# Attention and two mixtures of experts in one kernel: a different order of the first loads, scalings and casts

## What is computed

```
gamma = 1.0 - 2.0 ** (-5.0 - arange(H)); scale = 1.0 / sqrt(D)
for t in range(S):
    state = gamma * state + einsum('bhd,bhe->bhde', k[:, :, t], v[:, :, t])
    y[:, :, t] = scale * einsum('bhd,bhde->bhe', q[:, :, t], state)
```

```
h = x @ w_in                                       # 512 -> 2048
x = (max(h, 0) + alpha * min(h, 0)) @ w_out        # 2048 -> 512
```

## Time and profile before

| what | value |
|---|---|
| median of 3 runs | 981.75 us (981.25 to 981.96) |
| profiled execution, its own time | 981.86 us |
| its span, first to last instruction | 979.9 us |
| TensorE matmul busy | 956.0 us (98%) |
| VectorE, ScalarE, GpSimd busy | 577.8, 255.2, 239.2 us |
| mean granted TensorE clock | 0.998 |

### The profile page before, as it was taken

The page is one execution under the profiler, slowest core; times in us unless marked ns, Lnnn a source line. Parts: engine busy times, 40 slices in busy tenths (PEclk is TensorE's granted clock), DMA queues, the critical chain, the costliest instruction groups (busy, mean ns, idle before and its releaser), DMA issues.

```text
span 979.9 us, 16519 instructions
## 1 busy us (share of the span) xinstructions
PE 956.0 (98%) x5444; PEld 792.8 (81%) x5445; DVE 577.8 (59%) x1078; ACT 255.2 (26%) x404; POOL 239.2 (24%) x192
## 2 busy tenths in 40 slices
PE   8999999999999999999999999999999999999996
PEld 7888888888888888888887888878788788787785
DVE  4656589647964697469845987664333632423531
ACT  4222121112111111121111312332433533323531
POOL 4443123331433142414341224120000000000000
PEclk9999999999999999999999999999999999999999
DMA  8431392033002300140012123355331451423311
GB/s 287 166 131 55 119 386 101 0 115 101 0 0 86 128 0 0 47 146 1 1 44 93 70 87 110 105 169 220 129 130 52 181 225 43 170 82 116 113 41 53
DMA packets 27121, 100.47 MB, mean 103 GB/s; under 512 B 4383, under 2 KB 4767, under 8 KB 22448
## 3 DMA queue, kind: packets, MB, share of 16 engines
q1 hardware_dynamic: 19280, 80.90, 23.2%
q0 software_dynamic: 4336, 12.61, 3.3%
q10 hardware_dynamic: 3456, 6.32, 2.3%
HBM read 87.19 MB, written 24.20 MB: 114 GB/s over the span
## 4 chain that ended last, share of the span: by engine, by line
PE 90%; issue 3%; DVE 2%; ACT 2%; ACTq 1%; DMA 1%; SPq 0%; DVEq 0%; POOL 0%; POOLq 0%
PE bank L676 27%; PE bank L694 27%; PE bank L801 13%; PE bank L769 11%; PE bank L572 2%; PE bank L784 2%; PE bank L618 2%; PE bank L588 2%; ACT weights_split L1370 1%; PE bank L605 1%; PE bank L661 1%; DMA en_all<-in_qk 1%; DVE attention L887 1%; DVE en_all L1138 0%; ACT scratch L1399 0%
## 5 line engine op out<-in xcount | busy, mean ns | idle before, releaser
L676 PE MATMUL bank<-activations_split,weights_split 128*128 128x512 f32 x1152 | 277.6, 391 | 0.4 <-issue 0.4
L694 PE MATMUL bank<-weights_split,activations_split 128*128 128x512 f32 x1152 | 276.1, 389 | 0.0
L694 PEld LDWEIGHTS bank<-weights_split,activations_split 128*128 128x128 f32 x1152 | 216.1, 188 | 44.9
L676 PEld LDWEIGHTS bank<-activations_split,weights_split 128*128 128x128 f32 x1152 | 215.1, 188 | 45.9 <-issue 1.5
L1511 POOL TENSOR_TENSOR activations_split<-scratch,activations_split 128x512 fp32r<-128x512 f32 x84 | 116.9, 1391 | 327.2 <-ACT activations_split L1290 319.8
L1290 ACT CAST activations_split<-scratch 128x512 fp32r<-128x512 f32 x96 | 59.8, 623 | 412.1 <-DVE scratch L927 412.1
L801 PE MATMUL bank<-weights_split,activations_split 128*128 (+1 forms) x648 | 161.5, 398 | 2.8 <-issue 1.8
L769 PE MATMUL bank<-weights_split,activations_split 128*128 (+1 forms) x648 | 153.3, 391 | 0.1
L769 PEld LDWEIGHTS bank<-weights_split,activations_split 128*128 128x128 f32 x648 | 121.0, 188 | 25.2 <-issue 0.5
L801 PEld LDWEIGHTS bank<-weights_split,activations_split 128*128 128x128 f32 x648 | 117.8, 188 | 26.4 <-issue 2.6
L986 DVE SCALAR_TENSOR_TENSOR attention<-rows,en_all 128x512 f32<-128x512 f32 x140 | 135.0, 1005 | 0.0
(11 more groups left out here) (183 smaller groups left out, 667.1 us busy)
## 6 DMA issues: line engine op xcount, KB each, us to landing
attention<-in_w_exp SPq DMA_DIRECT2D x24, 1024.0 KB, 4.9
attention<-in_kv SPq DMA_DIRECT2D x43, 256.0 KB, 3.7
expert_rows<-in_pad_rows SPq DMA_DIRECT2D x8, 1028.0 KB, 18.4
en_all<-in_w_exp SPq DMA_DIRECT2D x8, 1024.0 KB, 7.2
rows<-in_w_mlp SPq DMA_DIRECT2D x14, 512.0 KB, 3.3
rows<-expert_rows ACTq DMA_DIRECT2D x24, 257.0 KB, 2.9
attention<-in_qk SPq DMA_DIRECT2D x12, 512.0 KB, 4.7
scratch<-in_qk SPq DMA_DIRECT2D x10, 512.0 KB, 3.7
```

The lines of the kernel that those rows point to most:

```text
L676: last = mm(H_ps[f % 2][:, :], win(a, kc, f), x[:, kc, :], start=(k == 0), stop=(k == 3 * KC - 1))
L694: last = mm(bank[j][:, :], x[f % 2][:, j * P:(j + 1) * P], wout(a, f), start=(f == 0 and a == 0 and part_ == "hi"), stop=(f == FB - 1 and ...
```

## The change

SP now issues the four q/k slabs directly behind the first masks, and then the weight slabs. The four v slabs and the mask rest are issued from ScalarE's queue, ahead of everything else that ScalarE does. The q of pair 1 is scaled on VectorE, between `masked(0, 0)` and `masked(0, 1)`, and announced by a semaphore of its own; GpSimd scales pairs 2 and 3 only. In chunk 0 each pair has a result bank of its own (banks 2, 1, 0, 3), so `values(0, 2)` and `values(0, 3)` no longer wait for an `x_low`. VectorE runs `masked(0, 3)` without an `x_low` behind it, and then `x_low(0, 2)` and `x_low(0, 3)`; `x_low(0, 1)` stays ahead of `masked(0, 3)`. ScalarE's order becomes `first_values(2)`, `first_values(3)`, `split_w(0)`, `x_high(0, 1)`, `x_high(0, 2)`, `x_high(0, 3)`. Ten dummies instead of twelve.

```diff
--- before.py
+++ after.py
@@ -257,8 +257,13 @@
 
     A_ps = pair[:, :].rearrange("p (h b c) -> p h b c", h=2, b=B)
     A0_ps = [[A_ps[:, 0], A_ps[:, 1]], [b3(6), b3(7)]]
+    Y_first = [b3(2), b3(1), b3(0), b3(3)]
     Y_ps, SU_ps, SU0_ps = [b3(2), b3(1)], b3(3, D), [b3(6, D), b3(7, D)]
     H_ps = [bank[4], bank[5]]
+
+    def Y_of(c, hp):
+        return Y_first[hp] if isinstance(c, int) and c == 0 else Y_ps[hp % 2]
+
     LG_ps = bank[7][:, 0:B * E].rearrange("p (b e) -> p b e", b=B)
     RK_ps = bank[6][:, 0:B * E].rearrange("p (b e) -> p b e", b=B)
     RK_last = bank[3][:, 0:B * E].rearrange("p (b e) -> p b e", b=B)
@@ -297,7 +302,7 @@
     s_vs_first, s_q_first, s_wlo_pool, s_zero, s_tau, s_masks_rest = sem("vs_first"), sem("q_first"), sem("wlo_pool"), sem("zero"), sem("tau"), sem("masks_rest")
     s_k_ld = [sem(f"k_ld{i}") for i in range(2)]
     s_v_ld = [sem(f"v_ld{i}") for i in range(3)]
-    s_v_first = sem("v_first")
+    s_v_first, s_q_second = sem("v_first"), sem("q_second")
     s_wld = [sem(f"wld{i}") for i in range(4)]
     s_whi, s_wlo = sem("whi"), sem("wlo")
     s_vs, s_qs, s_A, s_m, s_Yi, s_SU, s_Y, s_S, s_xh, s_xl = (
@@ -440,16 +445,9 @@
 
 
             sp.dma_start(C[:, :QD + P], consts[:, :QD + P]).then_inc(s_masks, 16)
-            load_qk(0, 0)
-            load_v(0, 0)
-            sp.dma_start(C[:, QD + P:MASKS], consts[:, QD + P:MASKS]).then_inc(s_masks_rest, 16)
-            load_qk(0, 1)
-            load_v(0, 1)
-            load_qk(0, 2)
-            load_v(0, 2)
-            load_qk(0, 3)
+            for hp in range(HP):
+                load_qk(0, hp)
             load_w(0)
-            load_v(0, 3)
             load_w(1)
             sp.dma_start(alpha_sb[:, :], alpha[:, :]).then_inc(s_small, 16)
             load_w(2)
@@ -557,8 +555,10 @@
                 first = isinstance(c, int) and c == 0
                 if first and hp == 0:
                     pe.wait_ge(s_q_first, due(s_q_first, 1))
+                elif first and hp == 1:
+                    pe.wait_ge(s_q_second, due(s_q_second, 1))
                 else:
-                    pe.wait_ge(s_qs, due(s_qs, u))
+                    pe.wait_ge(s_qs, due(s_qs, u - 1))
                 if not first:
                     pe.wait_ge(s_m, due(s_m, u))
                 elif hp >= 2:
@@ -610,12 +610,10 @@
                 pe.wait_ge(s_m, due(s_m, u + 1))
                 scaled(c, hp)
                 mixed = Am_first[hp % 2] if first else Am
-                if first and hp >= 2:
-                    pe.wait_ge(s_xl, due(s_xl, u - 1))
                 for b in range(B):
                     for hh in range(2):
                         cols = slice(hh * D, (hh + 1) * D)
-                        last = mm(Y_ps[hp % 2][cols, b, :], v_sb(c, hp)[:, b, cols], mixed[:, hh, b, :],
+                        last = mm(Y_of(c, hp)[cols, b, :], v_sb(c, hp)[:, b, cols], mixed[:, hh, b, :],
                                   start=first, stop=(first or b == B - 1))
                 last.then_inc(s_Y, 1)
 
@@ -722,7 +720,7 @@
                         x_transpose(0, 1)
 
             pe.wait_ge(s_zero, due(s_zero, 1))
-            for _ in range(12):
+            for _ in range(10):
                 mm(bank[0][:, 0:P], idle_in, idle_in, start=True, stop=True)
             scores(0, 0)
             values(0, 0, first=True)
@@ -878,7 +876,7 @@
             def x_low(c, hp):
                 u = 4 * c + hp
                 dve.wait_ge(s_xh, due(s_xh, u + 1))
-                ve.tensor_tensor(x_lo[:, hp, :].rearrange("p (b c) -> p b c", b=B), Y_ps[hp % 2],
+                ve.tensor_tensor(x_lo[:, hp, :].rearrange("p (b c) -> p b c", b=B), Y_of(c, hp),
                                  x_hi[:, hp, :].rearrange("p (b c) -> p b c", b=B).bitcast(f32),
                                  ALU.subtract).then_inc(s_xl, 1)
 
@@ -902,15 +900,23 @@
                           .then_inc(s_S, 1)
                 x_low(c, HP - 1)
 
-            def first_attention():
+            def second_query():
+                dve.wait_ge(s_masks_rest, due(s_masks_rest, 16))
+                dve.wait_ge(s_qk_ld[1], due(s_qk_ld[1], 16))
+                ve.tensor_tensor(qT(0, 1), qT(0, 1), qdecay[:, 1:2, :].broadcast_to([P, B, P]), ALU.mult).then_inc(s_q_second, 1)
+
+            def first_attention(between):
                 for hp in range(HP):
                     dve.wait_ge(s_A, due(s_A, hp + 1))
                     if hp >= 2:
                         dve.wait_ge(s_Y, due(s_Y, hp - 1))
                     masked(0, hp, A0_ps[hp % 2], Am_first[hp % 2])
-                    if hp:
+                    if hp == 0:
+                        between()
+                    elif hp < HP - 1:
                         x_low(0, hp - 1)
-                x_low(0, HP - 1)
+                for hp in range(HP - 2, HP):
+                    x_low(0, hp)
                 split_w(1)
 
             def mlp(c, router_c=None):
@@ -1101,7 +1107,7 @@
             dve.wait_ge(s_masks, due(s_masks, 16))
             dve.wait_ge(s_qk_ld[0], due(s_qk_ld[0], 16))
             ve.tensor_tensor(qT(0, 0), qT(0, 0), qdecay[:, 0:1, :].broadcast_to([P, B, P]), ALU.mult).then_inc(s_q_first, 1)
-            first_attention()
+            first_attention(second_query)
             dve.wait_ge(s_small, due(s_small, 16))
             low_done(dve, 0)
             low_done(dve, 1)
@@ -1267,7 +1273,7 @@
 
             def x_high(c, hp):
                 act.wait_ge(s_Y, due(s_Y, 4 * c + hp + 1))
-                se.copy(x_hi[:, hp, :].rearrange("p (b c) -> p b c", b=B), Y_ps[hp % 2]).then_inc(s_xh, 1)
+                se.copy(x_hi[:, hp, :].rearrange("p (b c) -> p b c", b=B), Y_of(c, hp)).then_inc(s_xh, 1)
 
             def attention(c):
                 for hp in range(HP):
@@ -1324,6 +1330,14 @@
                 act.wait_ge(s_rc, due(s_rc, CHOOSE * c))
                 se.activation(probs, diff, ACT.Exp).then_inc(s_exp, 1)
 
+            def load_first_v(hp):
+                act.dma_start(v_sb(0, hp), kv[bass.ds(0, 1), hp, :, 1].rearrange("o p (b n) -> p (o b) n", b=B))\
+                   .then_inc(s_v_first if v_sb(0, hp) is v_first else s_v_ld[hp % 3], 16)
+
+            load_first_v(0)
+            act.dma_start(C[:, QD + P:MASKS], consts[:, QD + P:MASKS]).then_inc(s_masks_rest, 16)
+            for hp in range(1, HP):
+                load_first_v(hp)
             act.wait_ge(s_zero, due(s_zero, 1))
             se.activation(nrm[:, 0:1], idle_in[:, 0:1], ACT.Copy, scale=1.0)
             act.wait_ge(s_masks, due(s_masks, 16))
@@ -1331,9 +1345,9 @@
             first_values(1)
             x_high(0, 0)
             first_values(2)
+            first_values(3)
+            split_w(0)
             x_high(0, 1)
-            split_w(0)
-            first_values(3)
             x_high(0, 2)
             x_high(0, 3)
             split_w(1)
@@ -1534,7 +1548,7 @@
                 if 0 < p < 16:
                     pool.sem_inc(s, p)
             pool.wait_ge(s_masks_rest, due(s_masks_rest, 16))
-            for hp in range(1, HP):
+            for hp in range(2, HP):
                 query_decay(0, hp)
 
             def split_w(n):
```

## The result

The changed kernel takes 983.62 us in the median of 15 executions (982.79 to 984.29), the kernel before 981.68 in 15 (981.01 to 983.88). The ratio is 1.0019, with a 95% interval of 1.0011 to 1.0027: slower by about 1.9 us. The forecast was 982.5 in a range of 980.9 to 984.5, with a chance of 0.77 for less than 0.2% (1.96 us) either way. The way there does not hold: what happened is, in part, two rivals together, B (the loads came sooner) and D (TensorE's clock), and the forecast's own mechanism did not decide.

The account below looks back on a forecast made before the run. The chain's order before hidden(0, 0) at 18.82 us was taken to decide, with gapless TensorE work behind. Start +0.64 and follow-up +0.13 made +0.77: 982.6 against the profiled execution, 982.5 against the median; range 980.9 to 984.5.

Parts of the forecast that it names:

- B: Rival for the startup loads: two queues improve the pace by 0.7 us or more, giving 980.9 to 982.0; chance 0.23.
- D: Rival for TensorE's clock: pauses and gaps keep it low at the start, +1.5 (983.3) to +5.4 (988.0 in sum); chance 0.16.
- the forecast's own mechanism: Startup: slab 0's cast ahead of x_high(0, 1) delays the first hidden group by 0.64 us; 982.0 to 982.9, chance 0.50.
- Pairing of transfers: Startup loads: transfers of the two queues alternate about one for one, so they land in pairs, then slab 0 alone.
- Pace of two queues: Startup loads: landings at equal KB stay near the old ones, 0.2 us sooner: slab 0 at 14.7, q/k 2 at 11.5.
- The other bound, 1.73: Startup loads: if two queues filled the slow stretch, everything would come 1.73 us sooner, slab 0 at 13.17.
- The cast of slab 0 decides: ScalarE: x_high(0, 1) waits for slab 0's cast until 15.80, later by 0.6 us than the path through q/k 2.
- the other branch gives 15.2: Path from q/k 2 landing at 11.5 through scores and values: x_high(0, 1) could start at 15.2, 3.73 us later.
- Ten dummies cost nothing, since q/k 0 isn't scaled by then: TensorE's start: ten dummies end at 5.53 instead of 6.42, before q/k 0 is scaled; cost 0.
- Follow-up of 0.13 at the second hidden group: hidden(0, 1) waits for slab 1's low part until 22.29 where TensorE wants it at 22.18; 0.13 with the hop.
- q 1 on VectorE, own result banks, issue time on ScalarE, table load: Startup side effects: q 1 and banks 0; ScalarE's issues about 2.2 us, then table load 1.28, done before v 0 arrives.
- TensorE without a gap from 18.82 us on: Main stream: from 18.82 us TensorE's matmuls run gapless, 2.72 us per group of 12, so only the start's shift counts.

Follow-up runs that it names:

- fourteen and five dummies: Changed kernel with fourteen dummies instead of ten, plus five more between the first scores and the first values: 982.00 us, ratio 0.9997.
- the reordered version with ten: Changed kernel, ten dummies, none between; masked(0, 3) ahead of x_low(0, 1), slab 1 cast behind x_high(0, 1), made low ahead of x_low(0, 3): 983.25 us, ratio 1.0014.

## Why the prediction came out as it did

- **Pairing of transfers**: right. Masks and v 0, q/k 0 and the mask rest, and so on, land in pairs; q/k 0 at 6.5, within 5.1 to 7.31.
- **Pace of two queues**: the term that was mis-sized. I took 0.2 us off the old landing at equal KB and measured 0.85 for slab 0 (14.05 for 14.9). The other bound, 1.73, was too far the other way. The tail's window, on which I leant, has other transfers in it and doesn't show the start. The third q/k slab came sooner as well: GpSimd works on it from 10.93, where the forecast's 11.5 with 0.17 to the start is 11.67.
- **The cast of slab 0 decides**: wrong as to this kernel. The step "the other branch gives 15.2" had TensorE at full clock. It came at 16.64, behind the low clock, and the cast was over at 15.1. With the clock kept up, cast and branch meet as the prediction has it (`x_high(0, 1)` directly behind the cast, at 14.77), and the wait behind it is 0.80 us. With the old loads, where v 3 comes late too, it is 2.34 us, and the 3.64 us of the prediction are found again.
- **Ten dummies cost nothing, since q/k 0 isn't scaled by then**: the step that failed. It looked at TensorE's path and not at its clock, which the text kept for rival D at 0.16. The pause was put at up to 1.3 us and was 1.81. The 1.3 doesn't follow from the prediction's own bounds: with q/k 0 at 7.31, and 0.15, 0.69 and 0.04 as it has them, the scores start at 8.19, 2.66 behind the dummies' 5.53. That wider pause would have been a reason to give D more. D priced the low clock at +1.5 or more; fourteen dummies alone take the changed kernel from 1.94 above its before (983.62 to 981.68) to 0.16 above its own (981.96 to 981.80), so the clock is worth 1.8 us, and what is left of the whole change is 0.16 where the forecast had 0.8.
- **Follow-up of 0.13 at the second hidden group**: right in kind. It is 0.30 in the changed kernel and 0.29 with the clock up, 0.02 when slab 1 is made ready earlier.
- **q 1 on VectorE, own result banks, issue time on ScalarE, table load**: nothing of them shows on the path. They weren't tried one by one.
- **TensorE without a gap from 18.82 us on**: the earlier trace rows shows it as far as they go. The earlier trace rows gives a tenth of the chain, some 98 us, to other things, most of it later. It didn't matter: a first down group 26.07 - 24.38 = 1.69 us later made the span 1.6 longer.

That the time landed in the range is luck: two errors met. The slab came sooner than forecast, and so would the other branch have at full clock, but the clock took more than that back. The forecast had a loss of 0.8 us by the cast and got one of 1.9 by the clock.

## What to carry to other kernels

When a change delays the first load, look at what TensorE does until then: fillers should reach to the first real matmul (twelve were too few here, fourteen were enough in ten of 11 executions), because a pause at the start can be paid several us later at the lower clock. An instruction moved forward on one in-order engine is safe only as long as what it waits for lands before everything behind it is wanted, so a load order and a cast order are one change and not two. And an earlier start of the main stream is worth only what its second step can follow.

## What the hardware showed beyond that

- The clock needn't fall in the pause itself. In the changed kernel TensorE pauses from 5.52 to 7.32, the group at 7.32 still runs at full pace, and the lower clock comes after it. Nor does work lift it at once: with ten dummies and five between, TensorE works without a break from 7.40 us on, and from 9.2 to 12.4 us the clock is at 0.50 all the same. The window of that kernel, with TensorE's busy time and then clock, DMA share and GB/s at the end:

```profile
9.20:12.40 3.20, 3.20 (x25) 2.65 (x23) 1.30 (x3) 0.85 (x2) 1.23 (x1) 0.50 1.04 418
```

- The mean granted clock doesn't tell such executions apart reliably. It is 0.994 to 0.997 in the changed kernel and 0.997 to 0.999 with fourteen and five dummies, but also 0.997 to 0.999 in the kernel before with four dummies, whose first scores take 2.08 us, and 0.999 in the slowest execution of the reordered version with ten (984.77). The durations of groups of the same shape are the surer sign.
- Two queues moved 331 GB/s from 2 to 9 us, where one moved 307 in the kernel before and 312 in the changed kernel with its loads on SP. Later there is no difference (407 to 409). The Trainium skill (DMA: Bandwidth & Descriptors, Issuing engines are not separate DMA queues) counts only issue time as saved. That may be the whole of it, since slab 0 was issued at 3.35 instead of 5.50; it wasn't separated. By the rule on packets in the Trainium skill (DMA: Bandwidth & Descriptors, Queues, rings and completion order), as the prediction worked it out, q/k 0 would not have waited for the mask rest. Here they landed together, q/k 0 at 6.5 and the mask rest at 1.19 + 5.4 = 6.6, so the row speaks for turns by single rows; no run tried it apart.

```profile
constants<-in_consts ACTq DMA_DIRECT2D x1, 192.0 KB, 5.4
```

- The price of sharing is at the front: the same 132 KB of masks take 3.8 us to land instead of 2.2, and q/k 0 5.3 instead of 3.8. That delay and the two dummies fewer opened the pause together: it is 0.77 us with the delay and twelve dummies, 0.25 with ten dummies and no delay, 1.81 with both.
